# Mixture-of-experts kernel: the share column goes out in four parts, the tile table is written beside the list, and the next pass's rows are read before the last results are written

## What is computed

```python
def reference(**kwargs):
    attn_out = _attn_ref(**attn_kwargs)          # B=2, S=3584, D=192
    x = attn_out.reshape(B * S, D)
    x = _moe_ref(x=x, **moe_kwargs)              # top 2 of 8 experts, hidden width 1024
    return _moe2_ref(x=x, **moe2_kwargs)         # top 1 of 8 experts, hidden width 1024

def _moe2_ref(x, w_gate, w1, w2):
    logits = x @ w_gate
    expert_idx = np.argmax(logits, axis=1)
    probs = softmax(logits)                      # written out in the reference
    gate_w = probs[np.arange(N), expert_idx]
    for e in range(E):
        mask = expert_idx == e
        h = np.maximum(x[mask] @ w1[e], 0.0)
        out[mask] = gate_w[mask, None] * (h @ w2[e])
```

## Time and profile before

| | us |
|---|---|
| median of 3 runs | 1204.32 (1201.09 to 1206.36) |
| the profiled execution's own time | 1202.42 |
| its span in the profile | 1200.1 |
| PE busy in the span | 1074.8 (90%) |
| DVE busy in the span | 789.8 (66%) |
| mean granted TensorE clock | 0.964 of full |

### The profile page before, as it was taken

The page is one execution under the profiler, slowest core; times in us unless marked ns, Lnnn a source line. Parts: engine busy times, 40 slices in busy tenths (PEclk is TensorE's granted clock), DMA queues, the critical chain, the costliest instruction groups (busy, mean ns, idle before and its releaser), DMA issues.

```text
span 1200.1 us, 28811 instructions
## 1 busy us (share of the span) xinstructions
PE 1074.8 (90%) x7844; PEld 1024.5 (85%) x7845; DVE 789.8 (66%) x1381; ACT 542.1 (45%) x1072; POOL 536.1 (45%) x658
## 2 busy tenths in 40 slices
PE   3962999999999999999999999998999797999995
PEld 2541898989999999898999999998989697999995
DVE  9998889897677545555585545556556854656652
ACT  2340444454543444466344434456654443554542
POOL 1000466555444544434454545555444434655552
PEclk9985899999999999999999999999999998999998
DMA  7152223234223333538535333246766732543510
GB/s 247 54 165 73 69 90 115 91 101 130 79 87 86 96 91 113 164 96 205 127 89 101 93 90 108 77 125 196 205 155 110 154 104 83 150 123 102 145 41 22
DMA packets 105621, 136.54 MB, mean 114 GB/s; under 512 B 33834, under 2 KB 83821, under 8 KB 105324
## 3 DMA queue, kind: packets, MB, share of 16 engines
q1 hardware_dynamic: 86124, 92.99, 28.8%
q0 software_dynamic: 19456, 43.07, 12.7%
HBM read 104.78 MB, written 34.57 MB: 116 GB/s over the span
## 4 chain that ended last, share of the span: by engine, by line
PE 60%; DVE 15%; DMA 9%; issue 8%; ACT 3%; POOL 2%; DVEq 1%; ACTq 1%; POOLq 1%; PEldq 0%; SPq 0%
PE ps_y L1607 17%; PE ps_y L1608 8%; DMA row<-x_rows,read_now 7%; PE ps_h L1552 5%; PE ps_h L1556 5%; PE ps_h L1562 5%; PE ps_h L1559 5%; PE ps_h L1553 5%; DVE prod L640 4%; PE ps_x L1541 2%; PE ps_y L1619 2%; PE ps_x L1542 2%; DVE h_lo L972 2%; DVE prod L652 1%; DVE prod L857 1%
## 5 line engine op out<-in xcount | busy, mean ns | idle before, releaser
L1607 PE MATMUL ps_y<-w_hl,h_hi 128*128 128x384 f32 x1344 | 404.4, 366 | 7.4 <-DVE h_lo L972 6.8
L972 DVE SCALAR_TENSOR_TENSOR h_lo<-ps_h,h_hi 128x512 fp32r<-128x512 f32 x404 | 259.9, 686 | 189.1 <-ACT h_hi L1309 179.2
L1608 PE MATMUL ps_y<-w_hl,h_lo 128*128 128x192 f32 x1344 | 337.6, 251 | 0.0
L1309 ACT ACTIVATE h_hi<-ps_h 128x512 fp32r<-128x512 f32 x370 | 202.8, 596 | 226.7 <-PE ps_h L1562 218.8
L512 POOL DMA_INDIRECT row<-x_rows,read_now x202 | 227.7, 1127 | 121.2 <-POOL read_now L508 85.8
L1607 PEld LDWEIGHTS ps_y<-w_hl,h_hi 128*128 128x128 f32 x1344 | 253.7, 189 | 10.6 <-DVE h_lo L972 10.5
L1608 PEld LDWEIGHTS ps_y<-w_hl,h_lo 128*128 128x128 f32 x1344 | 257.6, 192 | 0.0
L1552 PE MATMUL ps_h<-xa_hi,w1a_hi 128*128 128x256 f32 x672 | 196.6, 292 | 3.9 <-issue 2.6
L1556 PE MATMUL ps_h<-xa_lo,w1a_hi 128*128 128x256 f32 x672 | 191.2, 285 | 0.8 <-DVE xa_lo L954 0.8
L1553 PE MATMUL ps_h<-xa_hi,w1a_lo 128*128 128x256 f32 x672 | 190.3, 283 | 1.3 <-issue 1.3
L1562 PE MATMUL ps_h<-xb_lo,w1b_hl 128*128 128x256 f32 x672 | 190.8, 284 | 0.0
(11 more groups left out here) (206 smaller groups left out, 1611.7 us busy)
## 6 DMA issues: line engine op xcount, KB each, us to landing
w_raw<-in_moe_w_dram SPq DMA_DIRECT2D x32, 768.0 KB, 5.0
w1a_raw<-in_moe_w_dram SPq DMA_DIRECT2D x32, 512.0 KB, 3.5
w1b_raw<-in_moe_w_dram SPq DMA_DIRECT2D x64, 256.0 KB
x_rows<-tok SPq DMA_DIRECT2D x21, 384.0 KB, 7.1
x_pad<-in_x_dram SPq DMA_DIRECT2D x2, 2688.0 KB, 10.2
x_pad<-y_rows SPq DMA_DIRECT2D x14, 384.0 KB, 4.0
prod<-y_rows SPq DMA_DIRECT2D x14, 384.0 KB, 5.4
row<-x_rows,read_now POOLq DMA_INDIRECT x202
```

What stands on the lines that cost most here:

```text
L972: nc.vector.scalar_tensor_tensor(out=h_lo[:, i * GF:(i + 1) * GF, :], in0=ps_h[:, i, :].rearrange("p (f t) -> p f t", f=GF), scalar=0.0, i ...
L1309: act.activation(h_hi[:, i * GF:(i + 1) * GF, :], ps_h[:, i, :].rearrange("p (f t) -> p f t", f=GF), ACT.Relu).then_inc(h_hi_ready, 1)
L1607: nc.tensor.matmul(ps_y[:, u, 0:2 * D], h_hi[:, i, cols], w2_hl[b][:, f, :], start=(i == 0), stop=False)
L1608: last = nc.tensor.matmul(ps_y[:, u, 0:D], h_lo[:, i, cols], w2_hl[b][:, f, 0:D], start=False, stop=(i == FC - 1))
```

## The change

It has five parts:

1. `write_table` is parted in two. The four operations that make `tile_of`, `tile_mark` and `row_mark` stay where they were, as `give_rows`. The table itself is written by `place(q, 3)` at step `LIST`, ahead of the list; before pass 0, behind `mark_rows`.
2. `list_rows` makes `read_from` first and signals it with a new semaphore, `reads_listed`; `lists_ready` waits for that one. `write_to` and `found_ready` follow.
3. Before pass 0, `split_rows(0)` runs between the two last multiplications of `softmax_divide(1)`, where it stood behind both.
4. The share column is stored in four parts of 896 values, at steps `COUNT + 1` to `COUNT + 4`. Each waits for `y_ready` of the tile before.
5. In pass 2, `read_next_pass` stands ahead of `write_rows` where k is at least `LIST[2] - 1` = 14.

```diff
+        SHARE_PARTS = 4
+        assert all(LIST[p] - COUNT[p] >= SHARE_PARTS for p in (1, 2)) and TP % SHARE_PARTS == 0
...
-                    with sp.If(j == COUNT[p] + 1):
-                        sp.wait_ge(scales_made, q - C + 1)
-                        rows_of = x_rows[q].rearrange("(q t) d -> q t d", q=P)
-                        sp.dma_start(rows_of[:, :, XW:SCALED_W], share_sum[:, :].unsqueeze(2), allow_slow_non_contiguous=True)                            .then_inc(x_stored[q], 16)
+                    with sp.If(j > COUNT[p]):
+                        with sp.If(j <= COUNT[p] + SHARE_PARTS):
+                            sp.wait_ge(scales_made, q - C + 1)
+                            if in_tile:
+                                sp.wait_ge(y_ready, g0 + j + 1)
...
+                            t = bass.ds(part * (TP // SHARE_PARTS), TP // SHARE_PARTS)
+                            rows_of = x_rows[q].rearrange("(q t) d -> q t d", q=P)
+                            sp.dma_start(rows_of[:, t, XW:SCALED_W], share_sum[:, t].unsqueeze(2), allow_slow_non_contiguous=True)\
+                                .then_inc(x_stored[q], 16)
...
-                pool.wait_ge(found_ready, p + 1)
-                pool.wait_ge(x_stored[p], 16 * (2 * NB, *(2 * TP // COLS[q] + (q > 0) for q in range(PASSES - 1)))[p])
+                pool.wait_ge(reads_listed, p + 1)
+                pool.wait_ge(x_stored[p], 16 * (2 * NB, *(2 * TP // COLS[q] + SHARE_PARTS * (q > 0) for q in range(PASSES - 1)))[p])
...
+                if p == 2:
+                    with pool.If(k + 2 >= n):
+                        with pool.If(k >= LIST[p] - 1):
+                            read_next_pass(p, g0, n, k)
                 write_rows(p, g0, k)
                 if p == 2:
                     with pool.If(k + 2 >= n):
-                        read_next_pass(p, g0, n, k)
+                        with pool.If(k < LIST[p] - 1):
+                            read_next_pass(p, g0, n, k)
...
                 pool.wait_ge(routed, p + 1)
+                pool.wait_ge(found_ready, p + 1)
...
-            def softmax_divide(c):
+            def softmax_divide(c, between=None):
...
                     dve.wait_ge(done, 5 + i)
+                    if i == 1 and between is not None:
+                        between()
...
+                elif part == 2:
+                    give_rows(p, step, v)
                 else:
                     write_table(p, step, v)
...
+            def give_rows(p, step, v):
...
+            def write_table(p, step, v):
...
-                step(v.scalar_tensor_tensor(out=found_id[:, :], in0=found[:, :], scalar=float(S // 2 + c * S), in1=found_id[:, :],
+                v.scalar_tensor_tensor(out=read_from[p % 2][:, :], in0=found[:, :], scalar=float(S // 2), in1=found_id[:, :],
+                                       op0=ALU.add, op1=ALU.add).then_inc(reads_listed, 1)
+                step(v.scalar_tensor_tensor(out=found_far[:, :], in0=found[:, :], scalar=float(S // 2 + c * S), in1=found_id[:, :],
                                             op0=ALU.add, op1=ALU.add))
...
+                if j == LIST[p]:
+                    place(q, 3)
...
             for part in range(3):
                 place(0, part)
             mark_rows()
+            place(0, 3)
             list_rows(0)
-            softmax_divide(1)
-            split_rows(0)
+            softmax_divide(1, lambda: split_rows(0))
```

More of the change, by code:

```diff
@@ L200, in build @@
         found_ready = sem("found_ready")
+        reads_listed = sem("reads_listed")
         scales_made = sem("scales_made")
@@ L406, in store_columns, with side @@
                 sp.dma_start(rows_of[:, :, D:XW], tok[q % C][:, t, P:D]).then_inc(x_stored[q], 16)
-            def side(p, g0, j):
+            def side(p, g0, j, in_tile=True):
                 q = p + 1
@@ L419, in side @@
                 if 1 <= p:
-                    with sp.If(j == COUNT[p] + 1):
-                        sp.wait_ge(scales_made, q - C + 1)
-                        rows_of = x_rows[q].rearrange("(q t) d -> q t d", q=P)
-                        sp.dma_start(rows_of[:, :, XW:SCALED_W], share_sum[:, :].unsqueeze(2), allow_slow_non_contiguous=True)                            .then_inc(x_stored[q], 16)
+                    with sp.If(j > COUNT[p]):
[3 more added lines that the diff above has]
+                                sp.wait_ge(y_ready, g0 + j + 1)
+                            part = nc.s_assert_within(j - (COUNT[p] + 1), 0, SHARE_PARTS - 1,
+                                                      skip_runtime_bounds_check_because="side work runs at its own steps alone")
+                            t = bass.ds(part * (TP // SHARE_PARTS), TP // SHARE_PARTS)
+                            rows_of = x_rows[q].rearrange("(q t) d -> q t d", q=P)
+                            sp.dma_start(rows_of[:, t, XW:SCALED_W], share_sum[:, t].unsqueeze(2), allow_slow_non_contiguous=True)\
+                                .then_inc(x_stored[q], 16)
             def section(p, g0, e, s, nxt):
@@ L452, in experts @@
                         with sp.Fori(n, STEPS) as j:
-                            side(p, g0, j)
+                            side(p, g0, j, False)
             load_taps(0)
@@ L777, in give_places @@
                     step(v.tensor_reduce(pos[:, k, :], d_lane[:, :, :], AX, ALU.add))
-            def write_table(p, step, v):
+            def give_rows(p, step, v):
                 ks = slice(0, choices(p))
@@ L833, in list_rows @@
                     step(v.tensor_tensor(found[:, :], ps_found[:, 0:NA], found_1[:, :], ALU.add))
-                    step(v.tensor_scalar(found_1[:, :], found_1[:, :], 0.0, float(N), ALU.not_equal, ALU.mult))
                 else:
@@ L837, in list_rows @@
                 step(v.tensor_scalar(found_id[:, :], found[:, :], 0.0, -1.0, ALU.is_gt, ALU.mult))
-                step(v.scalar_tensor_tensor(out=found_id[:, :], in0=found[:, :], scalar=float(S // 2 + c * S), in1=found_id[:, :],
+                v.scalar_tensor_tensor(out=read_from[p % 2][:, :], in0=found[:, :], scalar=float(S // 2), in1=found_id[:, :],
+                                       op0=ALU.add, op1=ALU.add).then_inc(reads_listed, 1)
+                step(v.scalar_tensor_tensor(out=found_far[:, :], in0=found[:, :], scalar=float(S // 2 + c * S), in1=found_id[:, :],
                                             op0=ALU.add, op1=ALU.add))
-                step(v.tensor_scalar(found_far[:, :], found[:, :], 0.0, float(NOWHERE), ALU.is_equal, ALU.mult))
                 if layer == 0:
+                    step(v.tensor_scalar(found_1[:, :], found_1[:, :], 0.0, float(N), ALU.not_equal, ALU.mult))
                     step(v.tensor_tensor(found_far[:, :], found_far[:, :], found_1[:, :], ALU.add))
-                step(v.tensor_scalar(read_from[p % 2][:, :], found_id[:, :], -float(c * S), None, ALU.add))
-                v.tensor_tensor(write_to[p % 2][:, :], found_id[:, :], found_far[:, :], ALU.add).then_inc(found_ready, 1)
+                step(v.tensor_scalar(found[:, :], found[:, :], 0.0, float(NOWHERE), ALU.is_equal, ALU.mult))
+                v.tensor_tensor(write_to[p % 2][:, :], found[:, :], found_far[:, :], ALU.add).then_inc(found_ready, 1)
                 dve.wait_ge(found_ready, p + 1)
```

## The result

| | before | changed |
|---|---|---|
| median of 9 runs each | 1202.65 (1199.75 to 1207.23) | 1210.67 (1206.68 to 1211.90) |
| ratio, 95% interval | | 1.0058 (1.004 to 1.0076) |
| the profiled execution's own time | 1202.42 | 1211.27 |
| its span | 1200.1 | 1209.1 |
| mean granted clock | 0.964 | 0.959 |

The change makes the kernel slower by 0.6%: 7.0 us by the ratio, in which each run is set against those beside it, and 8.0 by the two medians.

A forecast was written before the change was run, and what follows sets the result against it. PE's work was taken to set the time, an edit paying only in PE's gaps. Terms +2.4 - 0.7 - 4.5 + 10.5 = +7.7 gave 1212, range 1202 to 1219 (the forecast's own 1208 to 1215).

The forecast's parts named there:

- The start: Before pass 0: PE starts later and DVE ends later than the rows' shift says; +2.4, from -1.2 to +2.4.
- The rows: Before pass 0: the first rows come with the last of expert 1's weights, at 122.3, 1.5 later than before.
- The split: Before pass 0: DVE still has the second last softmax multiplication to do when the rows come, ending 0.9 later.
- Passes 0 and 1: Table moves at no cost; in pass 1 the gap of 0.72 at 642.44 goes: -0.7, 0 at worst.
- Pass 2, tiles 12 to 14: Table leaves tile 12, tile 13's y waits less for the scatter, clock gains: -4.5, from -3.0 to -6.6.
- The scatter's 2.6: Pass 2: y of tile 13 keeps 1.0 of its 3.64 wait for tile 12's scatter, so -2.6.
- The clock's -0.8: Pass 2, behind the gap at 958.30: less of PE's busy 4.70 at clock 0.53; -0.8 of at most 2.0.
- The boundary: Passes 2 to 3: part four goes behind the last w2 load, delaying gathers, scatter and xa_lo: +10.5, +7 to +16.
- part four is in time: Rival at the boundary: part four lands by the middle of tile 16's `down`; -6.0 there, sum -8.8, 1195; chance 0.10.
- gathers slip past weights: Rival before pass 0: the gathers pass expert 1's weights; start -1.2, sum +4.1, 1208; chance 0.20.
- Small writes: Rival: part four takes the whole column's 9.5; boundary +15, tile 13's wait stays, sum about +16, 1220; chance 0.14.
- the column never held the scatter: Rival: w1 and w2 held it; tile 13 keeps its gap, sum about +11, 1215; chance 0.08.

## Why the prediction was right

The forecast, 1212 for 1210.67, came by its own mechanism, and its terms can be read one by one. It was +7.7 on the 1204.32 of three runs; measured were +7.0 by the ratio and +8.0 on 1202.65, the median of nine.

**The start, +2.4.** The rows, +1.5: PE's first transposes came 1.90 later, but DVE already ran 0.85 late in this execution before the first edited operation (`give_places` of 97.94 stood at 98.79), so +1.05. The last weight load landed at 122.3 (7.1 after 115.16) and PE started at 122.66, as the boundary's row had suggested. This execution was a mild one: from the end of the issue to PE's start it had 4.97, and the seven runs with the new start and the weights ahead of the rows had 4.8 to 5.8, 5.3 in the mean, which makes +1.4 of the +1.5 forecast. The split, +0.9: PE's transposes of `taps` are these, before and after.

```profile
138.49 0.33 PE L1471 MATMUL ps_x<-ident,taps 128*128 128x128 f32 x1 [0.48 <-ACT taps L1225]
```

```profile
141.29 0.33 PE L1497 MATMUL ps_x<-ident,taps 128*128 128x128 f32 x1 [0.48 <-ACT taps L1251]
```

They stand 17.73 and 18.63 behind the first transposes: +0.90. Sum +1.95 in this execution. The low end, -1.2, rested on gathers that slip past the weights, and the run with the weights moved shows that they don't.

**Passes 0 and 1, -0.7.** The gap at 642.44 is gone, and comes back with the whole column; in its place PE has none of 0.25 or more. What that did to the time can't be read, since the two executions drift by more.

**Pass 2, tiles 12 to 14, -4.5.** The table's 1.1 came (2.05 to 0.96). The scatter's 2.6 came as 2.5 (5.61 to 3.08), by way of ACT: y of tile 13 waits 1.29 for it and none for the scatter. Five executions with four parts had gaps of 2.83 to 3.08 there; the three with the whole column had 3.47, 5.61 and 6.16, so the term is somewhere from 0.4 to 3.3. The clock's -0.8 did not come in this execution. Windows of the same width behind the gap of 5.61 and at the third matmul of pass 3 (busy us by engine, then the granted clock, the DMA share and GB/s), before:

```profile
958.30:965.00 6.70, 6.70 (x36) 6.70 (x37) 4.75 (x7) 1.39 (x4) 3.07 (x5) 0.67 0.42 113
1002.95:1010.05 7.10, 7.10 (x44) 7.10 (x44) 1.56 (x3) 2.49 (x4) 4.08 (x5) 0.71 0.20 51
```

and after:

```profile
960.56:967.26 6.70, 6.70 (x32) 6.70 (x33) 4.36 (x6) 1.39 (x4) 3.05 (x5) 0.60 0.44 113
1014.92:1022.02 7.10, 7.10 (x38) 7.10 (x39) 1.56 (x3) 2.03 (x3) 2.52 (x5) 0.60 0.23 50
```

Behind that gap the granted clock was 0.60 against 0.67 over 6.70, a loss of 0.5 in place of the gain, so the term measured -3.1 here. One pair of executions doesn't decide this: behind the same gap the other four runs with four parts had 0.75 three times and 1.00 once (after a gap of 3.03), and the other two with the whole column 0.63 and 0.75. So a shorter gap may have spared PE some of the low level, 1.2 GHz, or not; the forecast's -0.8 is neither shown nor excluded.

**The boundary, +10.5.** From L to the third matmul, 7.15 became 16.41: +9.3. The clock adds 0.8 (0.71 to 0.60 over 7.10), which the forecast had at nothing; that isn't shown to be of the change, since the changed kernel run again had 0.76 there, and 16.6 to its third matmul. The steps: part four issued at L+1.8 (L+1.1); landed about L+5.1 (L+6.1), since w2 took 4.8 from 998.13, and the part came 0.7 behind it and not 1.5; transposes L+10.55 (L+11.4); y of tile 17 L+14.2 (L+15.1); xa_lo L+15.9 (L+17.2), 1.0 of table reads ahead of it and not 1.3.

**The sum.** +1.95 - 0.7 - 3.1 + 10.1 = +8.2, and +6.9 without the two readings of the clock, against +7.7 forecast and 7.0 (4.8 to 9.1) by the ratio. That it came within a microsecond is partly luck: the term of tile 13 alone spreads by more from execution to execution, and the boundary was forecast 1.2 too high. In the two profiled executions the changed one is 3.4 behind at the start of pass 1, 5.5 just before tile 13's `down` in pass 2, 2.7 at L, 12.0 at the third matmul of pass 3 and 9.0 at the end. The 2 us between the start of pass 1 and tile 13, and the 3 given back in pass 3, lie where the forecast had no cost; stretches of lower clock stand there (824 to 829 at 0.80 after, 1138 to 1147 at 0.77 and 0.84 before). They are of these executions, not shown to be of the change.

**The rivals.** That part four is in time (-6.0 at the boundary) is what one or two parts make true: -3.8 there by the rows, where the forecast had -3.5 and another -2.5 for the clock, of which the rows show 0.4 to 0.9 (0.76 and 0.83 for 0.71 over 7.10); the whole was -6 to -9 by the medians, where the rival had -8.8. That gathers slip past weights is excluded. Small writes do land sooner when they are smaller: 9.5 for the whole column, 6.2 for half of it, and part four 3.3. That the column never held the scatter is excluded by the runs with one and two parts.

One slip in its working changes nothing: the low bound of part four is L+3.6 (L+1.1 and 2.5), not L+3.8.

What stays open is by what rule the DMA engines let the weights go first and then mixed them with the rows, how much of the term of tile 13 is the clock, and how the rest of a ratio is made up where two sets differ by 0.002 for the same kernel (0.9925 and 0.9948 with two parts).

## What to carry to other kernels

When a transfer is cut into parts that go out at successive steps, look for who does the steps and what it waits for ahead of them: SP did the last section's steps only behind a weight load, and so the last quarter of 14 KB went out some 30 us after the third. The same reordering (reads ahead of writes) earned 3.8 with its condition met early and cost 3.3 with it met late; price a reordering by when the wait inside it ends. And a signal that releases bulk loads should not be moved onto a small urgent gather: ask what else hangs on a signal that is delayed. Moving the bulk loads behind the urgent gather is no free way out either: here the next gather was then held by them.

## What was not expected of the hardware

Two gathers of 128 rows each took 1.8 to 1.9 from the end of the issue to PE's start in the seven runs with nothing ahead of them, and 4.8 to 5.8 in the seven with four weight loads (some 1.8 MB in all) issued in the 4 us ahead. In the two looked at above, this was the data itself: with the weights ahead no packet of the rows moved before 119, with none ahead the first moved before 117.

A column of 4-byte values took 9.5, 6.2 and 3.3 to land for 3584, 1792 and 896 of them, each behind a load of w2, though the last at another place of the pass.

The granted clock over the 6.7 us behind the gap in front of tile 14 did not follow the length of the gap: 0.67, 0.63 and 0.75 behind gaps of 5.61, 6.16 and 3.47; 0.56 to 0.77 behind gaps of 3.87 to 4.59; 0.60, 0.75, 0.75, 0.75 and 1.00 behind gaps of 2.83 to 3.08.

And one kernel had medians 0.7% apart in three sets of runs, of which the first two, 0.3% apart, were on the same chip.
